# Attention and two dense layers on one core: the first matmul of both layers as a seven-product (Strassen) scheme, d_ff in two halves, attention in 128-query tiles

## The reference

```python
# q, k, v: 8 batches x 8 heads x 576 positions x 64
k_p = k.reshape(B, H, 72, 8, D).mean(axis=3)          # keys and values averaged over 8 positions
v_p = v.reshape(B, H, 72, 8, D).mean(axis=3)
scores = (1.0 / np.sqrt(D)) * np.matmul(q, k_p.transpose(0, 1, 3, 2))
scores = scores - np.max(scores, axis=-1, keepdims=True)
attn = np.exp(scores)
attn = attn / (np.sum(attn, axis=-1, keepdims=True) + 1e-09)
x = np.matmul(attn, v_p).transpose(0, 2, 1, 3).reshape(4608, 512)
h = x @ w_in1;  g = h * (1.0 / (1.0 + np.exp(-h)));       y = g @ w_out1      # 512 -> 2048 -> 512
h = y @ w_in2;  g = h * np.clip(h + 3.0, 0.0, 6.0) / 6.0; out = g @ w_out2
```

## Time and profile before

| | |
|---|---|
| time, median of 3 runs (lowest to highest) | 1819.33 us (1816.72 to 1820.5) |
| the profiled execution: its own time, and the span of its trace | 1817.3 us |
| mean granted TensorE clock | 0.992 of full speed |
| PE busy | 98% of the span, 11028 matmul records |
| DVE / ACT / POOL busy | 50% / 32% / 3% |

### The profile page before, as it was taken

The page is one execution under the profiler, slowest core; times in us unless marked ns, Lnnn a source line. Parts: engine busy times, 40 slices in busy tenths (PEclk is TensorE's granted clock), DMA queues, the critical chain, the costliest instruction groups (busy, mean ns, idle before and its releaser), DMA issues.

```text
span 1817.3 us, 28625 instructions
## 1 busy us (share of the span) xinstructions
PE 1777.1 (98%) x11028; PEld 1610.7 (89%) x11028; DVE 911.0 (50%) x1543; ACT 589.8 (32%) x1291; POOL 54.2 (3%) x44
## 2 busy tenths in 40 slices
PE   4999999999999999999999999999999999999999
PEld 3899999999999999999999888888888888888887
DVE  5774663754745736647445443434343433334343
ACT  3644443444444434444446211111111111111111
POOL 3400000000000000000003000000000000000000
PEclk7999999999999999999999999999999999999999
DMA  5530120200300202003105101010101010101000
GB/s 130 147 79 27 27 53 28 60 21 28 79 28 19 61 28 59 21 28 79 43 1 167 63 1 47 1 47 1 46 0 46 0 46 0 46 8 39 20 4 23
DMA packets 87572, 74.99 MB, mean 41 GB/s; under 512 B 40364, under 2 KB 64940, under 8 KB 87468
## 3 DMA queue, kind: packets, MB, share of 16 engines
q1 hardware_dynamic: 87468, 73.41, 14.6%
HBM read 54.53 MB, written 18.87 MB: 40 GB/s over the span
## 4 chain that ended last, share of the span: by engine, by line
PE 97%; DVE 1%; issue 1%; DMA 1%; ACT 1%; SPq 0%
PE acc L430 15%; PE acc L431 15%; PE acc L432 15%; PE hidden L430 11%; PE hidden L432 11%; PE hidden L431 11%; PE att L431 5%; PE att L432 5%; PE att L430 5%; PE att L480 2%; PE att L497 1%; PE att L498 1%; PE att L453 1%; DMA stage<-in_moe_w_in_dram 1%; DVE p_sb L1014 0%
## 5 line engine op out<-in xcount | busy, mean ns | idle before, releaser
L430 PE MATMUL hidden<-x_hi,win_hi 128*128 128x288 f32 (+1 forms) x1312 | 425.0, 324 | 11.5 <-issue 9.1
L432 PE MATMUL hidden<-x_hi,win_lo 128*128 128x288 f32 (+1 forms) x1312 | 419.2, 320 | 0.0
L431 PE MATMUL hidden<-x_lo,win_hi 128*128 128x288 f32 (+1 forms) x1312 | 415.6, 317 | 0.0
L430 PE MATMUL acc<-g_hi,wout_hi 128*128 128x288 f32 x1024 | 310.7, 303 | 0.0
L432 PE MATMUL acc<-g_hi,wout_lo 128*128 128x288 f32 x1024 | 302.4, 295 | 0.0
L431 PE MATMUL acc<-g_lo,wout_hi 128*128 128x288 f32 x1024 | 302.3, 295 | 0.0
L770 ACT ACTIVATE g_hi<-u 128x512 fp32r<-128x512 f32 x144 | 91.1, 633 | 636.6 <-DVE u L981 636.6
L430 PEld LDWEIGHTS hidden<-x_hi,win_hi 128*128 128x128 f32 x1312 | 249.0, 190 | 27.0 <-issue 13.8
L431 PEld LDWEIGHTS hidden<-x_lo,win_hi 128*128 128x128 f32 x1312 | 250.1, 191 | 12.9
L432 PEld LDWEIGHTS hidden<-x_hi,win_lo 128*128 128x128 f32 x1312 | 248.4, 189 | 13.2
L948 DVE TENSOR_TENSOR g_lo<-g_raw,g_hi 128x288 fp32r<-128x288 f32 x256 | 118.2, 462 | 219.4 <-ACT g_raw L738 217.9
(11 more groups left out here) (118 smaller groups left out, 2286.9 us busy)
## 6 DMA issues: line engine op xcount, KB each, us to landing
q_raw<-in_q_dram SPq DMA_DIRECT2D x48, 192.0 KB, 3.9
...
x_raw<-first_layer_t SPq DMA_DIRECT2D x9, 1024.0 KB, 5.2
out_dram<-o_stage SPq DMA_DIRECT2D x36, 256.0 KB, 2.1
stage<-in_moe_w_in_dram SPq DMA_DIRECT2D x32, 256.0 KB, 3.4
stage<-in_moe_w_out_dram SPq DMA_DIRECT2D x32, 256.0 KB, 2.7
...
```

The costliest lines, as they stand in the source:

```text
L430: nc.tensor.matmul(dst, s_hi, m_hi, start=start and i == 0, stop=False)
L431: nc.tensor.matmul(dst, s_hi, m_lo, start=False, stop=False)
L432: last = nc.tensor.matmul(dst, s_lo, m_hi, start=False, stop=stop and i == n - 1)
```

## The change

Tokens go in blocks of 512 through both layers, and d_ff in two halves of 1024, so that there are four passes (layer 1 half 0, layer 1 half 1, layer 2 half 0, layer 2 half 1) of 9 blocks, 36 steps. Only the weights of one pass are on the chip; those of the next are loaded, summed, rounded and split at its end. Passes 0 and 2 write a partial output to DRAM (`partial`); passes 1 and 3 read it back (`y_part`) and add it.

The first matmul of a step takes the hidden columns in 4 pairs p of 256, and computes the 256x512 result of a pair from a 512-deep product as 2x2 blocks by seven products instead of eight (the form of Strassen's scheme with 15 additions). The sums of weight blocks are made by POOL once per pass (`sums`: four tensor_tensor in a chain per pair), the sums of x blocks by DVE once per step (`sum_x`), and the sums of products by the accumulation in psum, by an ACT copy (`copy_p1`) and by four DVE additions per pair (`chain`, `finish_h`). A product is 6 matmuls of 128x256. Chunk a of a pair is four products (24 matmuls), chunk b three (18).

The second matmul follows as 32 units (j, f), where j is one of four output blocks and f one of 8 hidden blocks of the pass: 3 matmuls of 128x512. There are two psum banks `acc` instead of four, so that unit (2, 0), at place U+16, waits until bank 0 has been read. A place is a position in the step: 0 to 7 are the chunks, U = 8 is the first unit, END = 40 is behind the last.

Attention is computed in plain fp32 in 5 tiles of 128, 128, 128, 128 and 64 queries per batch, with its results going through DRAM (`attended_t`); the attention of batch s + 1 stands in step s of pass 0. POOL pools keys and values head by head (16 per batch, two slots `kv_stage`); before, DVE did so. ACT's queue issues the loads of q and the stores of x. All loops are written out.

```diff
-PLAN = {0: [("kt",)], 1: [("qt", 0)], 2: [("s", 0)], 3: [("qt", 1)], 4: [("s", 1)], 5: [("qt", 2)],
...
+CHUNKS = [("a", 0), ("a", 1), ("b", 0), ("b", 1), ("a", 2), ("a", 3), ("b", 2), ("b", 3)]
+UNITS = [(0, f) for f in range(6)] + [(1, f) for f in range(6)] + [(0, 6), (0, 7), (1, 6), (1, 7)] \
+    + [(2, f) for f in range(8)] + [(3, f) for f in range(8)]
+U = len(CHUNKS)
+END = U + len(UNITS)
+EVAC_AT = [U + 13, U + 15, U + 23, U + 31]
...
+PLAN_NEXT = {1: [("pt", -2)], 2: [("pv", -2)], 3: [("pt", -1)], 4: [("pv", -1), ("kt",)], 5: [("qt", 0)], 6: [("s", 0)],
+             7: [("qt", 1)], U: [("s", 1)], U + 2: [("qt", 2)], U + 4: [("s", 2)], U + 6: [("exp", 0, 3)],
+             U + 11: [("pt", 0)], U + 13: [("pv", 0)], U + 15: [("pt", 1)], U + 16: [("pv", 1)], U + 18: [("pt", 2)],
+             U + 20: [("pv", 2)], U + 21: [("qt", 3)], U + 22: [("s", 3)], U + 24: [("qt", 4)], U + 26: [("s", 4)],
+             U + 29: [("exp", 3, 5)]}
...
+def next_at(s):
+    return END if s in (0, 1) else U + 21 if s < B - 1 else U + 12
...
+                layer, cols = ps // 2, ps % 2 * HF + p * 2 * P
+                src = w_in_rows[layer][:, :, cols:cols + 2 * P]
...
+                        sp.wait_ge(w1_split, 4 + (ps - 1) * 8 + 2 * (p - 1))
+                    elif ps == 1:
+                        sp.wait_ge(x_stored, 16 * (TILES - FIRST))
+                        sp.wait_ge(kv_pooled, 2 * H * (B - 1))
+                    else:
+                        sp.wait_ge(w1_split, 4 + (ps - 1) * 8)
+                    sp.dma_start(w1_raw[:, p % 2], src).then_inc(w1_loaded[p % 2], 16)
...
+            def load_x(s):
+                ps, blk = divmod(s, NB)
+                sp.wait_ge(x_split, 4 * s)
+                if ps < 2:
...
+            for s in range(STEPS):
+                ps, blk = divmod(s, NB)
+                if ps == 0 and s + 1 < B:
+                    for n in range(H + 2 * H * s, min(H + 2 * H * (s + 1), 2 * H * (B - 1))):
+                        load_kv(n)
+                if ps and blk == 0:
+                    load_w2(ps)
+                if ps % 2:
+                    load_part(s)
+                late = ps == 0 and s < B
...
-                for c in range(CT):
-                    sp.dma_start(q_raw[:, c], q_rows[0, 0, c]).then_inc(first_q[c], 16)
-                sp.dma_start(v_first[:], v_rows[0]).then_inc(v_loaded, 16)
-            def load_kv(rows, which, b):
-                for j in range(NK):
...
+            def product(dst, p, stationary, moving, first):
+                s_hi, s_lo = stationary
+                m_hi, m_lo = moving
+                for i in range(2):
+                    nc.tensor.matmul(dst, s_hi[i], m_hi[i], start=first and i == 0, stop=False, skip_group_check=True)
+                    nc.tensor.matmul(dst, s_hi[i], m_lo[i], start=False, stop=False, skip_group_check=True)
+                    last = nc.tensor.matmul(dst, s_lo[i], m_hi[i], start=False, stop=i == 1, skip_group_check=True)
+                return last
...
+            def chunk_a(s, p):
...
+                        pe.wait_ge(w1_split, 4 + (ps - 1) * 8 + 2 * p + 2)
+                if p == 0:
+                    pe.wait_ge(x_split, 4 * s + 2)
+                if n >= 2:
+                    pe.wait_ge(xy_read, n - 1)
+                    pe.wait_ge(h_done, n - 1)
+                x, y = xy[p % 2][:, :HB], xy[p % 2][:, HB:]
+                z, w = zw[p % 2][:, :HB], zw[p % 2][:, HB:]
+                product(x, p, w_block(p, 0, 0), x_block(0, 0), True)
+                product(y, p, w_sum(p, 1), x_sums(1), False).then_inc(a_done, 1)
+                product(w, p, w_sum(p, 0), x_sums(0), True)
+                product(z, p, w_block(p, 0, 1), x_block(0, 1), False).then_inc(a_done, 1)
+            def chunk_b(s, p):
+                n = s * NPAIR + p
+                if p == 0:
+                    pe.wait_ge(x_split, 4 * s + 4)
+                x = xy[p % 2][:, :HB]
+                z, w = zw[p % 2][:, :HB], zw[p % 2][:, HB:]
+                pe.wait_ge(u2_done, n + 1)
+                product(x, p, w_block(p, 2, 0), x_block(2, 0), False).then_inc(x_done, 1)
+                pe.wait_ge(c22_done, n + 1)
+                product(w, p, w_block(p, 2, 1), x_sums(2), False)
+                product(z, p, w_sum(p, 2), x_block(2, 1), False).then_inc(zw_done, 1)
...
+            def unit(s, j, f):
+                ps, blk = divmod(s, NB)
+                if blk == 0 and j < 2:
+                    pe.wait_ge(w2_split, ps * NF + f + 1)
+                if j < 2 and f % 2 == 0:
+                    pe.wait_ge(g_split, s * NPAIR + f // 2 + 1)
+                if f == 0 and NK * s + j >= 2:
+                    pe.wait_ge(acc_read, NK * s + j - 1)
+                dst = acc[j % 2][:]
...
+            def round_g(s, p):
+                n = s * NPAIR + p
+                act.wait_ge(uh_done, n + 1 - 2 * NB * NPAIR)
+                nc.scalar.activation(g_hi[:, p], g_raw[:, p % 2], ACT.Copy).then_inc(g_rounded, 1)
...
+            def round_w1(ps, p):
+                raw, sums_ = w1_source(ps, p)
+                act.wait_ge(w1_summed, 4 * (ps * NPAIR + p) + 4)
+                if ps:
+                    act.wait_ge(zw_done, NPAIR * (ps * NB - 1) + p + 1)
+                nc.scalar.activation(w1r_hi[:, p], raw, ACT.Copy).then_inc(w1_rounded, 1)
+                nc.scalar.activation(w1s_hi[:, p], sums_, ACT.Copy).then_inc(w1_rounded, 1)
...
+            def sum_x(s):
+                b11, b12, b21, b22 = x_blocks()
+                t3, t2 = (x_sum[:, i].rearrange("p (c n) -> p c n", c=2) for i in range(2))
+                n = 4 * s
+                if s:
+                    dve.wait_ge(x_loaded, 16 * s)
+                else:
+                    dve.wait_ge(first_x_copied, FIRST)
+                    dve.wait_ge(first_x_kept, 2)
+                nc.vector.tensor_tensor(t3, b22, b12, ALU.subtract).then_inc(x_summed, 1)
+                dve.wait_ge(x_summed, n + 1)
...
+            for s in range(STEPS):
+                ps, blk = divmod(s, NB)
...
+                        if place in (3, 4, 7, U):
+                            swish_rest(s, {3: 0, 4: 1, 7: 2, U: 3}[place])
+                        if place in (2, 3, 6, 7):
+                            swish_first(s, CHUNKS[place][1])
+                            finish_h(s, CHUNKS[place][1])
+                        if place == 4:
+                            split_g(s, 0)
+                        if place in (0, 1, 4, 5):
+                            chain(s, CHUNKS[place][1])
+                        if place == 5:
+                            split_g(s, 1)
+                        if place == U:
+                            split_g(s, 2)
+                            split_g(s, 3)
+                    if blk == NB - 1 and ps + 1 < PASSES and place in (U + 1, U + 4, U + 7, U + 10):
+                        split_w1(ps + 1, (place - U) // 3)
+                    if ps % 2 and place in EVAC_AT:
+                        evacuate(s, EVAC_AT.index(place))
```

More of the change, by code:

```diff
@@ new lines, in transpose_p, with values @@
+            def transpose_p(tile, banks):
+                rows = ROWS[tile % CT]
+                for g in range(2):
+                    for h in range(GH):
+                        last = nc.tensor.transpose(banks[g][:SP, h * P:h * P + rows], p_sb[:rows, tile % 3, GH * g + h, :],
+                                                   ident[:rows, :rows])
+                    last.then_inc(pt_done, 1)
+            def values(src, tile, bank):
+                rows = ROWS[tile % CT]
+                for h in range(H):
+                    half = slice(h % 2 * D, (h % 2 + 1) * D)
+                    last = nc.tensor.matmul(bank[half, h // 2 * P:h // 2 * P + rows], v_pool[:, h, :], src[:, h, :rows],
+                                            start=True, stop=True)
+                last.then_inc(pv_done, 1)
@@ L756, in copy_out @@
[L756 to L774 removed]
+                    rows = ROWS[t % CT]
@@ L794, in attend_first, with exp, copy_p @@
+                def exp(c):
+                    rows = ROWS[c]
                     act.wait_ge(first_s_read, 2 * c + 2)
[L795 to L797 removed]
+                    nc.scalar.activation(p_sb[:rows, c % 3], p_sb[:rows, c % 3], ACT.Exp, scale=float(D) ** -0.5 / POOL)\
+                        .then_inc(exp_done, 1)
+                def copy_p(c):
```

1484 lines of the change are left out of this document (714 added, 770 removed), and 6 rows, old and new, of tables (BANKS, PLAN).

## The result

The changed kernel takes 1985.3 us (median of 4, 1981.4 to 1987.0) against 1818.0 for the kernel before, measured beside it: the ratio is 1.092, with a 95% interval of 1.090 to 1.093. It is 167 us slower.

The account below looks back on a forecast made before the run. PE's instruction intervals bound the kernel before (98% busy). Work, head and tail of 1706 plus waits and clock, 23 + 45 + 23 + 47 + 61 + 40, gave 1945, or 1947 us at the median; range 1850 to 2037.

Parts of the forecast that it names:

- blocks 1 and 2: Steps 0 and 1: x loads behind the last store, leaving PE idle 11.5 us each, 23 together.
- scores' bank, steps 2 to 6: Attention: PE's transpose waits for a bank whose reads stand behind x's sums on DVE; 45 us in all.
- step 0 and small waits of pass 0: First values wait for V pooled head by head and first w2, 15 us (5 to 30); other waits 8.
- ends of passes: Reads of acc stand behind new weights' splitting and x's sums, delaying unit (2, 0): 47 us over three ends.
- g_lo in layer 2, a step: Unit (0, 4) wants pair 2's g_lo at 2.8 us, PE sees it at 5.3: 2.5 in each of 18 steps.
- waits of passes 1 to 3 besides their ends: Waits for g_lo (45 us), the output's read in pass 3 and 0.75 late in pass 1: 61 with roundings.
- clock: PE's clock falls after waits: 25 us for eleven long waits, 15 for about half of 18 short ones; 40.
- Half of them hidden is 1850: Case where half of the waits from long blocks are hidden behind PE's work: 1850 us, chance 0.13.
- rival 1: Long blocks on other engines are hidden; block, pass and their clock waits go, leaving 61 and 23: 1790 us, chance 0.12.
- Rival 2: A 256-column product matmul costs what 288 columns do (0.1325 us), 90 us more: 2037, chance 0.11.
- Rival 3: All 18 layer 2 waits drop the clock, POOL slows DVE, step 0 hits its bound: 2001; 0.11 with rival 4.
- rival 4: Sums eat the saved product: cover for chunk b fails by 0.4 us in 144 chunks: 2005; 0.11 with Rival 3.

Follow-up runs that it names:

- experiment 2: Changed kernel with only x's sums and rounding in steps 7 to 34 moved behind the reads of outputs 0 and 1 (U+12 to U+16): 1945.2 us.
- experiments 1: Changed kernel with only PE's order of units of outputs 0 and 1 changed, so g_lo of pair 2 is wanted 2.8 us later: 1980.6 us.
- experiment 3: Changed kernel with both the new order of units and x's sums moved to U+16 in steps 7 to 34: 1887.6 us.
- experiment 12: Kernel with all reordering edits combined (1786.0 us), its seven products replaced by 12 matmuls of 128x512 per hidden block: 1791.7 us.

## Why the prediction was right, point by point

The measured values are worked out from the starts of PE's instructions in the timeline (a step runs from its first product to the next step's; the clock's price is the sum of what intervals at the lower level exceed 0.120 or 0.227 by, after the head; attention's is what steps 3 to 6 are longer than 41.94 by, less their waits and the clock's price).

It gave 1947 us, with 1850 to 2037 as the range; 1985 lies within, also within the forecast's own 1905 to 1990, and slower had 0.83. Its sum of 1945 stands against 1979.5 for the profiled execution. By its steps:

| term | predicted | measured |
|---|---|---|
| products, 6048 | 711 (0.1175) | 726 (0.120) |
| second matmul, 3456 | 808 (0.2337) | 784 (0.227) |
| head to the first product | 67 | 67.5 |
| attention of a batch | 16.5 | 19.9 to 20.2, changeovers within |
| blocks 1 and 2 | 23 | 12.2 + 11.9 |
| scores' bank, steps 2 to 6 | 14.5, 2 x 9.9, 2 x 5.5 | 11.9, 2 x 8.9, 2 x 4.8 |
| step 0 and small waits of pass 0 | 15 + 8 | 21.5 + 13 |
| ends of passes | 15.4, 16.4, 15.6 | 16.1, 17.3, 14.5 |
| g_lo in layer 2, a step | 2.5 | 2.4 |
| waits of passes 1 to 3 besides their ends | 61 | 61 |
| clock | 40 | 43 |

- The bound: it held. PE's work fell, as worked out, and PE's waits made the time: 207 us of them behind the head and 43 of clock, where 199 and 40 were forecast. The places were the named ones, and each followed from three orders and the durations in rows of before: g_lo of pair 2, forecast as seen at 5.3 and wanted at 2.8, is seen at 5.3 and wanted at 2.9 in the timeline shown above. PE busy is 87% where it said near 90, the granted clock 0.947 where it said 0.96.
- Mis-sized, too low: attention, and with it most of what the sum lacks: 25 of 34 us in seven batches. The sum has no price for the changes between attention's and the feed's matmuls, some 20 in a step; that the difference lies there is likely and wasn't taken apart. The small waits of pass 0 are 12 over the forecast, and step 0's low clock costs 7. The waits also cost about 8 more than their length, some 0.2 to 0.3 in every step that has one.
- Left out, without harm to the sum of 61: in step 9 the late x (5.3, experiment 2). In steps 18 and 27 g_lo is waited for 4.9 and 4.7 instead of 2.4: there POOL splits the new second weights, and DVE's L936 takes 2.2 to 2.3 us beside it, 1.22 alone.
- Mis-sized, too high: the second matmul (24) and the scores' bank (45 against 39). The former hides that the products cost 15 more than forecast; that the total is only 1.7% low owes something to luck.
- "Half of them hidden is 1850" is a slip: the terms that rival 1 takes away are 23 + 45 + 47 + 40 = 155, and half of them gone is 1870.
- Clock: about half of the 18 waits for g_lo were to drop it, and nine did, at 1.5 to 1.7 each where nothing else falls in: those of steps 18, 19, 26 to 30, 33 and 35. Which ones is not settled by the wait: it is 2.38 in steps 19 and 20 alike, and the granted clock behind it is 0.65 (1207.2 to 1212.0 us) and 1.00 (1253.5 to 1258.3); the steps are 46.27 and 44.61 us. In experiment 2, with the same waits, it fell in 19, 20 and 21 of the steps 19 to 25, here in 19 alone. So the half was a guess that came out, and what one row shows ("a wait of 2.8 dropped the clock") was too simple as a rule. A fall costs 1.7, as taken.
- The sum treated the waits as terms to add. For the time of this kernel that does no harm, as the chain passes through all of them; for what an edit would bring it fails (experiments 1, 2 and 3: 8, 44 and 100).
- Rival 1 (the blocks hidden, 1790) failed for this order. With all blocks moved the kernel takes 1786; that the numbers are so near is chance, since the rival keeps the 61 and 23 of waits and the moved blocks take most of those away too.
- Rival 2 failed (0.120, not 0.1325). Rival 3 had the clock fall behind all 18 waits (nine), and rival 4 failed: chunk b's waits for its sums are 0.3 us each, in steps 18 and 27 alone, and the ordinary steps of experiment 3 have no wait at all.
- By the Trainium skill ("Back-to-back issue gap" in TensorE: Matmul & The Clock Gate) the gap of an isolated matmul of N columns is N/2.4 + 2.5 ns, 109 for 256 columns and 216 for 512. The trace has 120 and 227 for matmuls that follow each other, 11 ns more at both widths.
- The sentence on which all hangs, that the products save PE time: 726 for what 512 columns would do in 784. Only 58 us in 36 steps, and by experiment 12 the sums take about 50 of them back.
